# Attention with three heads under way in threefold buffers, exponentials over two banks and value remainders on GpSimd

## The reference

```
mask = q_assign[:, :, :, None] == k_assign[:, :, None, :]
scores = scale * np.matmul(q, k.transpose(0, 1, 3, 2))
scores = np.where(mask, scores, -1000000000.0)
scores = scores - np.max(scores, axis=-1, keepdims=True)
attn = np.exp(scores)
attn = attn / (np.sum(attn, axis=-1, keepdims=True) + 1e-09)
return np.matmul(attn, v).astype(np.float32)
```

## Time and profile before

| | |
|---|---|
| median of three runs | 753.01 us (751.97 to 754.56) |
| the profiled execution | 753.77 us |
| its span in the trace | 752.1 us |
| TensorE busy | 703.3 us (94% of the span) |
| VectorE busy | 462.1 us (61%) |
| ScalarE busy | 347.2 us (46%) |
| GpSimd busy | 282.8 us (38%) |

### The profile page before, as it was taken

How to read it: one execution, slowest core, us unless ns; L and a number is a source line. 1 busy time by engine, 2 the same in 40 slices (tenths; PEclk the granted TensorE clock), 3 DMA queues, 4 the chain that set the end, 5 groups by cost and what they waited for, 6 DMA issues and landing times.

```text
span 752.1 us, 17337 instructions
## 1 busy us (share of the span) xinstructions
PE 703.3 (94%) x5949; PEld 581.0 (77%) x5958; DVE 462.1 (61%) x916; ACT 347.2 (46%) x682; POOL 282.8 (38%) x341
## 2 busy tenths in 40 slices
PE   8899899999999999888999999989999999999996
PEld 4577678777777777664798999955799999999995
DVE  6788888888888888847454665427623442634421
ACT  3287777777777777663304332303221232321300
POOL 4066666666666665550131221300213221312211
PEclk9899999999999999999999999999999999999998
DMA  8111111111111111982565999446354646662100
GB/s 255 33 33 47 39 42 45 42 43 42 42 42 43 43 38 24 377 321 85 178 242 201 354 331 349 151 156 255 106 188 159 231 162 222 261 232 97 45 28 29
DMA packets 45969, 105.49 MB, mean 140 GB/s; under 512 B 5459, under 2 KB 11603, under 8 KB 45936
## 3 DMA queue, kind: packets, MB, share of 16 engines
q1 hardware_dynamic: 36352, 87.60, 33.3%
q0 software_dynamic: 4544, 12.70, 5.3%
q10 hardware_dynamic: 5040, 4.77, 2.0%
HBM read 87.64 MB, written 13.11 MB: 134 GB/s over the span
## 4 chain that ended last, share of the span: by engine, by line
PE 49%; DVE 3%; DMA 2%; issue 1%; ACT 0%; POOL 0%; POOLq 0%; SPq 0%; DVEq 0%
PE hT_ps_layer L1136 25%; PE y_ps_layer L1149 6%; PE y_ps_layer L1153 6%; PE y_ps_layer L1156 6%; PE x_turn_layer L1123 2%; DMA x<-x_mid 1%; PE hT_ps_layer L1065 1%; PE hT_ps_layer L1063 1%; PE x_turn_layer L1053 1%; DVE row_one_hot_layer L965 0%; DMA x_tile_layer<-x_src,token_to_read_layer 0%; PE hT_ps_layer L1078 0%; DMA x_mid<-y_out_layer,y_token_layer 0%; PE count_ps_layer L1053 0%; PE rank_ps_layer L1053 0%
## 5 line engine op out<-in xcount | busy, mean ns | idle before, releaser
L1136 PEld LDWEIGHTS hT_ps_layer<-xT_layer,w 128*128 128x128 f32 x1664 | 189.7, 192 | 3.2 <-DVE xT_layer L998 1.2
L1136 PE MATMUL hT_ps_layer<-xT_layer,w 128*128 128x128 f32 x1664 | 190.1, 275 | 0.5 <-issue 0.5
L346 POOL TENSOR_TENSOR probs_lo<-probs,probs_hi 128x384 f16<-128x384 f32 x160 | 147.4, 950 | 29.7 <-ACT probs_hi L306 29.7
L887 ACT ACTIVATE hT_hi_layer<-hT_ps_layer 128x512 fp32r<-128x512 f32 x52 | 31.1, 597 | 239.4 <-PE hT_ps_layer L1136 239.4
L467 DVE TENSOR_REDUCE max_halves<-turn 128x1 f32<-128x384 f32 x192 | 99.8, 554 | 31.4 <-PE turn L565 26.9
L305 ACT ACTIVATE probs<-scores 128x384 f32<-128x384 f32 x192 | 98.1, 511 | 29.0 <-PE scores L586 26.4
L306 ACT ACTIVATE probs_hi<-scores 128x384 f16<-128x384 f32 x192 | 99.3, 517 | 0.0
L1025 DVE SCALAR_TENSOR_TENSOR hT_lo_layer<-hT_ps_layer,hT_hi_layer 128x512 fp32r<-128x512 f32 x52 | 34.7, 689 | 88.4 <-ACT hT_hi_layer L887 77.4
L565 PE MATMUL turn<-kB,qB 96*128 96x384 f32 x192 | 78.3, 422 | 10.1 <-DVE kB L461 6.2
L1200 POOL DMA_INDIRECT out_dram<-y_out_layer,y_token_layer x16 | 19.7, 1234 | 146.9 <-DVE y_out_layer L1036 146.9
L882 ACT ACTIVATE w_hi<-w 128x1024 fp32r<-128x1024 f32 x64 | 62.4, 1047 | 26.5 <-issue 26.5
(11 more groups left out here) (215 smaller groups left out, 1138.5 us busy)
## 6 DMA issues: line engine op xcount, KB each, us to landing
w<-in_moe_w_dram SPq DMA_DIRECT2D x32, 2048.0 KB, 9.5
w<-in_v_dram ACTq DMA_DIRECT2D x4, 768.0 KB, 5.7
qk_raw<-in_q_dram SPq DMA_DIRECT2D x16, 192.0 KB, 2.8
qk_raw<-in_k_dram SPq DMA_DIRECT2D x16, 192.0 KB, 2.8
qB<-qA SPq DMA_DIRECT2D x16, 192.0 KB, 2.7
kB<-kA SPq DMA_DIRECT2D x16, 192.0 KB, 3.1
x_src<-x SPq DMA_DIRECT2D x2, 1536.0 KB, 13.4
x_mid<-x SPq DMA_DIRECT2D x2, 1536.0 KB, 15.8
```

The lines of the kernel that those rows point to most:

```text
L346: nc.gpsimd.tensor_tensor(p_lo[slot][:, half], probs[slot][:, half], p_hi[slot][:, half], ALU.subtract).then_inc(p_lo_pool, 1)
L1136: t = nc.tensor.matmul(hp[n][:, i * P:(i + 1) * P], W1[par][:, c, f * P:(f + 1) * P], xT[:, c, :], start=(c == 0), stop=(c == CD - 1))
```

## The change

Three heads are under way in buffers of three (`raw`, `qA`, `kA`, `qB`, `kB`, the parts of v), with loops unrolled by three; `q_features`, `k_features` and `masks` are down to one buffer. The `turn` banks are used in a new order (turn_a, maxima, turn_m, turn_b). The first score tiles of head s+1 are issued at the end of step s. One exponential covers both banks. GpSimd subtracts 768 columns at a time; `v_lo` goes to GpSimd, for which ScalarE also scales v in place. VectorE writes the intermediate one-hot values as bf16, and does the division of head s-1 at the start of step s. Before the first maxima, step -1 turns head 1.

```
+    NB = 3
+    raw = [sb(f"qk_raw{i}", [P, 2, T * D], F32) for i in range(NB)]
+    natq = sb("q_features", [P, T, 2 * D], F32R)
+    natk = sb("k_features", [P, T, 2 * D], F32R)
...
-    def run(eng, step, pairs_after=1):
-
-        step(-1, 1)
-        step(0, 0)
-        step(1, 1)
-        with eng.Fori(1, HEADS // 2 - pairs_after) as j:
-            step(2 * j, 0)
-            step(2 * j + 1, 1)
-        for s in range(HEADS - 2 * pairs_after, HEADS):
-            step(s, s % 2)
+    def run(eng, step, rounds):
+
+        step(-1, 2, -1)
+        step(0, 0, 0)
+        with eng.Fori(0, rounds) as j:
+            step(3 * j + 1, 1, j)
+            step(3 * j + 2, 2, j)
+            step(3 * j + 3, 0, j + 1)
+        for s in range(3 * rounds + 1, HEADS):
+            step(s, s % NB, s // NB)
...
+            def exps(i, kt):
+                slot = kt % RING_P
+                p_lo_taken(act, i - 1 if kt < RING_P else i, (kt - RING_P) % T)
+                wait(act, pv_hi_done, T * i + kt - RING_P + 1)
+                act.wait_ge(scored[kt % 2], (T // 2) * i + kt // 2 + 1)
+                for p in (probs, p_hi):
+                    nc.scalar.activation(p[slot][:].rearrange("p (n c) -> p n c", n=2), sc[kt % 2][:, :, 0:HALF],
+                                         ACT.Exp, scale=SCALE).then_inc(probs_ready, 1)
...
+                if c:
+                    exps(s, 0)
+                if b:
+                    evac_b(s + 1, (r + 1) % NB)
+                if a:
+                    evac_a(s + 2, (r + 2) % NB)
+                if c:
+                    exps(s, 1)
+                if b and not first:
+                    split_v(s + 1, (r + 1) % NB)
+                if c:
+                    exps(s, 2)
+                if has(s, 3):
+                    hi(s + 3, r, k + 1)
+                if c:
+                    exps(s, 3)
+                    exps(s, 4)
+                if b:
+                    evac_m(s + 1, (r + 1) % NB)
                 if first:
                     split_v(0, 0)
-                if has(s, 1):
-                    b, m = use_m(s + 1, not has(s, 2))
-                    act.wait_ge(turned[b], m + 1)
-                    nc.scalar.activation(QB[1 - par][ROWS_MASK:ROWS_B, :], turn_h[b][0:M_PARTS, 0:S], ACT.Copy).then_inc(turn_free[b], 1)
-            run(act, step)
+                if c:
+                    exps(s, 5)
...
             def rest(i, kt):
                 slot = kt % RING_P
                 wait(pool, pv_done, T * i + kt - RING_P + 1)
-                for n in range(2):
-                    half = slice(n * HALF, (n + 1) * HALF)
-                    pool.wait_ge(probs_ready, 4 * (T * i + kt) + 2 * n + 2)
-                    nc.gpsimd.tensor_tensor(p_lo[slot][:, half], probs[slot][:, half], p_hi[slot][:, half], ALU.subtract).then_inc(p_lo_pool, 1)
+                pool.wait_ge(probs_ready, 2 * (T * i + kt) + 2)
+                nc.gpsimd.tensor_tensor(p_lo[slot][:], probs[slot][:], p_hi[slot][:], ALU.subtract).then_inc(p_lo_pool, 1)
+
+            def split_v(i, r):
+                pool.wait_ge(v_hi_done, 2 * i + 2)
+                nc.gpsimd.tensor_tensor(v_lo[r][:], v_of(i), v_hi[r][:, :, 0:D], ALU.subtract).then_inc(v_lo_done, 1)
...
+                c = has(s, 0)
                 if c:
                     rest(s, 0)
-                if a:
-                    lo_k(s + 2, par)
-                if c:
                     rest(s, 1)
                 if c and not (isinstance(s, int) and s == 0):
                     add_up(s - 1)
                 if c:
-                    for kt in range(2, T - 1):
-                        rest(s, kt)
-            run(pool, step)
+                    rest(s, 2)
+                if has(s, 3):
+                    lo(s + 3, r)
+                if c:
+                    rest(s, 3)
+                if has(s, 1):
+                    split_v(s + 1, (r + 1) % NB)
+                if c:
+                    rest(s, 4)
...
+                link(nc.vector.tensor_tensor(eqt[:], eq[:], tie_b[:].unsqueeze(1).to_broadcast([P, 2 * T, C]), ALU.mult))
+                link(nc.vector.tensor_reduce(topt[:], eqt[:], AX.X, ALU.max))
+                nc.vector.tensor_tensor(maskb[:, :, 0:C], eqt[:, 0:T, :], wide(topt[:, 0:T], T), ALU.is_equal).then_inc(mask_steps, 1)
+                nc.vector.tensor_tensor(maskb[:, :, 2 * C:3 * C], eqt[:, T:2 * T, :], wide(topt[:, T:2 * T], T), ALU.not_equal).then_inc(mask_steps, 1)
...
+            def rest(i):
+
+                slot = (T - 1) % RING_P
+                dve.wait_ge(pv_done, T * i + T - RING_P)
+                dve.wait_ge(probs_ready, 2 * T * i + 2 * T)
+                nc.vector.tensor_tensor(p_lo[slot][:], probs[slot][:], p_hi[slot][:], ALU.subtract).then_inc(p_lo_dve, 1)
...
+                if not (isinstance(s, int) and s < 1):
+                    out(s - 1, (r - 1) % NB)
...
+                    maximum(s + 1, (r + 1) % NB)
                 if first:
                     v_power()
-                    split_v(0, 0)
+                if has(s, 2):
+                    masks(s + 2)
                 if has(s, 0):
-                    kt = T - 1
-                    slot = kt % RING_P
-                    dve.wait_ge(pv_done, T * s + kt - RING_P + 1)
-                    for n in range(2):
-                        half = slice(n * HALF, (n + 1) * HALF)
-                        dve.wait_ge(probs_ready, 4 * (T * s + kt) + 2 * n + 2)
-                        nc.vector.tensor_tensor(p_lo[slot][:, half], probs[slot][:, half], p_hi[slot][:, half], ALU.subtract).then_inc(p_lo_dve, 1)
-                    dve.wait_ge(pv_done, T * s + T)
-                    link = link_from(dve, out_steps, OUT_STEPS * s)
-                    bc = lambda a: a.unsqueeze(2).to_broadcast([P, T, D])
-                    link(nc.vector.scalar_tensor_tensor(out=denom[:, 0, :], in0=pv_o[:, :, D:D + 1].rearrange("p t o -> p (t o)"), scalar=EPS,
-                                                        in1=none[par][:], op0=ALU.add, op1=ALU.add))
-                    link(nc.vector.reciprocal(denom[:, 1, :], denom[:, 0, :]))
-                    link(nc.vector.tensor_scalar(denom[:, 0, :], none[par][:], v_scale[:, 3:4], None, ALU.mult))
-
-                    wait(dve, x_done, s)
-                    link(nc.vector.scalar_tensor_tensor(out=o_attn[:], in0=pv_o[:, :, 0:D], scalar=v_down, in1=bc(denom[:, 1, :]),
-                                                        op0=ALU.mult, op1=ALU.mult))
-                    nc.vector.tensor_tensor(o_mean[:], pv_s.unsqueeze(1).to_broadcast([P, T, D]), bc(denom[:, 0, :]), ALU.mult).then_inc(out_steps, 2)
+                    rest(s)
                 if has(s, 2):
-                    masks(s + 2, par)
-            run(dve, step)
+                    evac_b(s + 2, (r + 2) % NB)
+            run(dve, step, 4)
...
+            def scores(i, r, kt):
+                if isinstance(i, int) and i == 0 and kt == 0:
+                    pe.wait_ge(v_topped, QUARTERS + 3)
+                wait(pe, probs_ready, 2 * (T * i + kt - 1))
+                for part in range(2):
+                    if part == 1 and kt == 0:
+                        b, m = use_m(i)
                         pe.wait_ge(turn_free[b], m + 1)
-                    lhs, rhs = ((KA[par][:], QA[par][:]), (KB[par][0:ROWS_B, :], QB[par][0:ROWS_B, :]))[part]
+                    lhs, rhs = ((KA[r][:], QA[r][:]), (KB[r][0:ROWS_B, :], QB[r][0:ROWS_B, :]))[part]
                     for n in range(2):
                         m = nc.tensor.matmul(sc[kt % 2][:, n, 0:HALF], lhs[:, kt * P:(kt + 1) * P], rhs[:, n * HALF:(n + 1) * HALF],
                                              start=(part == 0), stop=(part == 1))
-                        if part == 1:
-                            m.then_inc(scored[kt % 2], 1)
-
-            def sum_v(i, par):
-
-                pe.wait_ge(v_hi_done, i + 1)
+                m.then_inc(scored[kt % 2], 1)
...
+                if c and not (isinstance(s, int) and s == 0):
+                    weigh_lo(s - 1, (r - 1) % NB, T - 1)
                 if a:
-                    assign(s + 2, par)
+                    turn_a(s + 2, 0)
+                if c:
+                    scores(s, r, 2)
+                if a:
+                    turn_a(s + 2, 1)
+                if c:
+                    sum_v(s, r)
+                    weigh_hi(s, r, 0)
+                if a:
+                    turn_a(s + 2, 2)
+                    turn_a(s + 2, 3)
+                if b:
+                    maxima(s + 1, rb, kb, 0)
+                if c:
+                    scores(s, r, 3)
+                    weigh_hi(s, r, 1)
+                    weigh_lo(s, r, 0)
+                if b:
+                    maxima(s + 1, rb, kb, 2)
+                if a:
+                    assign(s + 2, ra, 0)
+                if b:
+                    maxima(s + 1, rb, kb, 4)
+                if c:
+                    scores(s, r, 4)
```

(34 more changed lines are left out.)

404 lines of the change are left out of this document (179 added, 225 removed).

## The result

The change made the kernel slower: 831.38 us median of four runs (827.55 to 835.92) against 753.56 us (751.97 to 754.56), a ratio of 1.1037 with a 95% interval of 1.0977 to 1.1097. Medians here are over all executions, and ratios leave out those more than 1.5% above the fastest of the same kernel. The forecast was 805 us in a range of 775 to 832, so the median lies 0.6 us inside the range's upper end. The direction and the chain of waits were right; the lost clock was much too small in the sum.

What follows compares the result with a forecast made beforehand. VectorE was the closer bound, with TensorE also waiting; the new order's waits make a head 20.85 us, 22.1 with GpSimd, 22.4 with the clock. 491.0 plus 14 heads (313.6) gives 805 us, range 775 to 832.

Steps and rivals of the forecast that it cites:

- The waits of the order: TensorE's waits per head: `turn_m` about 2 us, parts 0.6, masks 1, `sum_v` 0.5, tile 1 1.2; head 20.85 without GpSimd.
- GpSimd's block: Before M, VectorE's small steps with two SBUF inputs wait for GpSimd's subtraction, taking a head from 20.85 to 22.1 us.
- the last small step: Last of VectorE's seven small maximum steps, ending at M: issued at 20.7, ending at 22.1 us behind GpSimd's last subtraction.
- the rival in which the scalings wait too: Scalings and casts among VectorE's small steps also wait for GpSimd: head 23.2 us with the clock, 816 us; chance 0.13.
- A double subtraction: GpSimd's 768-wide subtraction, four between tile 1's exponentials and M: between 1.5 and 1.76 us each, taken as 1.76.
- I add 0.3 a head: Clock price for TensorE idling ahead of every M, one drop a head at 0.3 us: 22.1 becomes 22.4 us.
- The upper bound of 2 us: Most that a lower clock could cost a head, about half of 4.5 us of matmuls between M and 11.0.
- the rival with the halved clock: The clock halves for most of a head's sparse part: 2 us a head, 24.1 to 24.4, 829 to 833 us; chance 0.09.
- The forecast's own 795 to 815: Range of the 805 us case, from M of head 0 at +0 to +4 and doubles of 1.5 to 1.76; chance 0.42.
- M of head 0: End of head 0's last small maximum step: 35.6 us after 33.4, because step -1 turns head 1 first.
- The tail: From M of head 14 to the end of the value parts: kept at 34.8 us.
- the 1.5 us that I took off the first and last head: Of 14 heads, the first has no division before it (-0.5), the last no q, k pieces on GpSimd (-1.0).

Runs made afterwards that it cites:

- the filler run: Changed kernel plus zero matmuls on TensorE, seven ahead of `turn_m`'s wait and two ahead of the wait for the masks: 836.55 us, ratio 1.11.
- The two reorderings: Changed kernel with tile 1's exponentials ahead of the q and k copies, and TensorE's and ScalarE's work around `turn_m` reordered: 782.33 us, ratio 1.0385.
- clearing GpSimd: The 782 us version with GpSimd's queue reordered and its q and k remainders held back until the small maximum steps are done: 769.11 us, ratio 1.0207.
- the dose doubled: The 782 us version with one more 128x768 GpSimd subtraction, into a tile nobody reads: 810.48 us, ratio 1.0761.
- the version of 767 us: The 778.24 us version (769 us version, exponentials and `sum_v` reordered) with GpSimd's q and k remainders held back until the masks are made: 767.43 us, ratio 1.0172.
- the first reordering: Changed kernel with ScalarE's exponentials of tile 1 ahead of its four copies of q and k: 798.39 us, ratio 1.06.
- the port runs: Four runs on where GpSimd and VectorE meet, varying GpSimd's queue, an added subtraction and the division's place: 769.11, 810.48, 829.62 and 828.04 us.
- One kernel, executed six times: The 767 us version with each exponential taken one bank (384 columns) at a time: 776.92 us median of six, ratio 1.0153.

## Why the prediction was right in direction and short in size

*The waits of the order: right.* The forecast named `turn_m`, the parts, the masks, `sum_v` and tile 1's exponentials, 20.85 us a head without GpSimd. At full clock the head of the filler run is 22.43 with 0.77 at L477 and 0.5 at the division (L499: 0.73 instead of 0.23), so about 21.2 without them. The two reorderings brought back 49 us, and clearing GpSimd 13 more. That these waits carry the loss of a full-clock head is shown: with the reorderings of the two exponential tiles, of `turn_m`'s surroundings and of `sum_v`, and with GpSimd held off at the masks too, such a head is back at 18.79.

*GpSimd's block: the rule right, the step wrong, the size small.* I had the last small step, with two SBUF inputs, wait until 21.9. It was the second, with one input: 0.92 to 1.52 us instead of 0.17, to the end of GpSimd's instruction, and with the dose doubled the third as well (1.72). That is the mechanism of the rival in which the scalings wait too (816 us). Steps with two SBUF inputs wait as well (0.94 and 1.49 instead of 0.26), a reduction does not (L476 at 182.95 in the changed kernel, 0.17). The Trainium skill's *SBUF — State Buffer*, section "Who interferes with whom", has all three: `tensor_scalar` may take the shared pair, two SBUF inputs contend, `tensor_reduce` never does. The rows agree with it. A double subtraction took 1.65, and 1.60 from start to start, where I took 1.76. So GpSimd ended sooner, and in ten of the 16 heads the second step met nothing. In the changed kernel the block cost 4.7 us; my sum had 1.25 a head, 17 us.

*The clock: the step that failed.* "I add 0.3 a head" priced a drop by the kernel before, where six heads had one between them, and took over its price. The upper bound of 2 us, on which the rival with the halved clock rested (0.09), is nearer to what happened. Of the 76.5 us that the 14 heads grew, the order's waits at full clock explain (21.2 - 18.82) x 14 = 33, the block 5, and the remaining 38, 2.7 a head, go with the clock (0.81 instead of 0.99). They are what is left over, not measured by themselves. At a mean of 0.81 a head of 24.3 us has some 9 us at half clock (2 x 0.19 x 24.3), not one window. By the slopes above (3.2 to 6.5 us for each 0.01) the clock of the whole execution (0.983 before, 0.905 after) would be worth 25 to 51 us, an estimate from other orders of work. So what came is the forecast's order with the clock rival, whose 829 to 833 us hold the median. The forecast's own 795 to 815 missed it. That the wide range held it by 0.6 us is partly luck: a block that I had 13 us too large made up for a third of what the clock lacked.

What makes the clock fall is open. In the version of 767 us eleven heads of the same instructions, 18.8 us each, ran at 0.96 to 1.00, and two, 23.8 us each, at 0.74. The seven fillers before `turn_m` raised the mean clock and shortened nothing. From the changed kernel over the first reordering to both, the clock rose as the waits shrank (0.905, 0.933, 0.965), but that it is the waits that lower it is argued, not shown.

*The smaller terms.* M of head 0 was forecast at 35.6 and came at 35.9. The masks took 2.4 us from M (2.8). The tail was 37.9 instead of 34.8: its clock was 0.87, the old one's 0.95. The experts kept 420.45. Against the profiled 835.9 us the error is 31: the clock's 38 in place of 4 (+34), the block's 5 in place of 17 (-13), order waits of 2.4 instead of 2.0 a head (+5), the 1.5 us that I took off the first and last head (+1.5), and the tail (+3).

## What to carry to other kernels

When a change lets an engine wait longer in every turn of a loop, price those waits and ask what the clock is in a turn after the change. Here, by the account above, each us of wait took about one more with it (33 + 5 of waits, 38 left for the clock), and the rows of the kernel before could not show that, since it ran at 0.99. Move long GpSimd instructions away from short VectorE steps on the path, above all from one-input steps with everything in SBUF; reordering GpSimd's queue and holding it back by a semaphore of VectorE's was worth 13 us of 782, and nothing in the changed kernel, where the meeting only moved. Ask of each instruction what it would meet at its new place: `v_lo` of 1 us on VectorE took 2 there and cost 3.2 a head.

## What the runs showed of the hardware that I had not expected

- A TENSOR_SCALAR of six f32 elements, SBUF to SBUF, waited up to 1.73 us for a GpSimd subtraction of two SBUF operands. Beside the same subtraction a reduction (0.17), a RECIPROCAL (0.19) and a two-input step with one operand in PSUM (0.17) took their usual times, and so did a copy out of PSUM (0.95) beside a 384-wide one.
- GpSimd waits too: 1.54 instead of 1.00 us for a 384-wide subtraction, 1.92 instead of 1.65 for a 768-wide one, behind a two-input VectorE instruction that was issued first.
- On GpSimd a 768-wide f32 subtraction took 1.65 us where two of 384 had taken 1.76; on ScalarE a 768-wide exponential took 0.82 us and was 0.69 apart, where two of 384 were 0.78.
- One kernel, executed six times on one chip, spread over 37 us with the granted clock, while the kernel before stayed within 5 us beside it; beside the port runs one of its seven executions took 808 us at 0.814.
